# Attention values with the exponentials stationary and V moving, in a kernel of chunk-selected attention and routed experts

## The reference

```python
ub = np.sum(np.maximum(q[:, :, :, None, :] * k_min[:, :, None, :, :], q[:, :, :, None, :] * k_max[:, :, None, :, :]), axis=-1)
ub = np.where(causal, ub, -1000000000.0)
top_chunks = np.argsort(ub, axis=-1)[..., -top_k:]
scores = scale * np.matmul(q, k.transpose(0, 1, 3, 2))
...
mask = sel & (pos[:, None] >= pos[None, :])
scores = np.where(mask, scores, -1000000000.0)
attn = np.exp(scores - np.max(scores, axis=-1, keepdims=True))
attn = attn / (np.sum(attn, axis=-1, keepdims=True) + 1e-09)
out = np.matmul(attn, v)
...
logits = x @ w_gate
expert_idx = np.argmax(logits, axis=1)
for e in range(E):
    ...
        keep = np.argpartition(-gw, capacity)[:capacity]
        tok_idx = tok_idx[keep]
    h = np.maximum(x[tok_idx] @ w1[e], 0.0)
    out[tok_idx] = gate_w[tok_idx, None] * (h @ w2[e])
```

## Time and profile before

| what | value |
|---|---|
| runs | 266.33, 266.83, 269.99 us; median 266.83 |
| profiled execution | 266.53 us |
| its span, first to last instruction | 264.8 us |
| granted clock of PE over the span | 1.00 (the 2.4 GHz level) |
| busy PE, DVE, ACT, POOL | 256.2, 213.2, 149.6, 211.3 us |
| pairs 0 to 15 and what leads up to them | up to about 222 us of the span |

### The profile page before, as it was taken

How to read it: one execution, slowest core, us unless ns; L and a number is a source line. 1 busy time by engine, 2 the same in 40 slices (tenths; PEclk the granted TensorE clock), 3 DMA queues, 4 the chain that set the end, 5 groups by cost and what they waited for, 6 DMA issues and landing times.

```text
span 264.8 us, 9133 instructions
## 1 busy us (share of the span) xinstructions
PE 256.2 (97%) x3824; PEld 164.4 (62%) x3824; DVE 213.2 (81%) x582; ACT 149.6 (56%) x227; POOL 211.3 (80%) x280
## 2 busy tenths in 40 slices
PE   7799999999999999999999999999999999989993
PEld 7366566666666566666665666656665657676763
DVE  6886696778989988867889889899999998983332
ACT  2295656565667564647584546564856665873320
POOL 6068889998999899897989898979899971726872
PEclk9999999999999999999999999999999999999999
DMA  9989989999799989997999999999799996941782
GB/s 147 189 145 149 235 225 261 228 187 224 125 208 180 209 145 195 173 219 125 215 160 215 171 190 164 215 162 324 142 207 184 328 212 142 165 103 40 136 167 91
DMA packets 148616, 48.34 MB, mean 183 GB/s; under 512 B 131583, under 2 KB 138870, under 8 KB 148512
## 3 DMA queue, kind: packets, MB, share of 16 engines
q1 hardware_dynamic: 135504, 28.73, 54.1%
q0 software_dynamic: 9936, 18.64, 38.6%
q10 hardware_dynamic: 3136, 0.39, 1.0%
HBM read 57.03 MB, written 11.01 MB: 257 GB/s over the span
## 4 chain that ended last, share of the span: by engine, by line
PE 91%; DVE 3%; ACT 2%; DMA 1%; issue 1%; ACTq 1%; POOL 0%; DVEq 0%
PE OB L637 28%; PE SC L546 27%; PE SC L567 7%; PE OB L1395 4%; PE MM L673 4%; PE SC L1369 4%; PE MM L650 3%; PE OB L721 2%; PE MM L474 2%; PE SC L474 2%; PE MM L513 2%; DMA qn<-in_q_dram 1%; ACT EXB L576 1%; PE MM L712 1%; PE MM L982 1%
## 5 line engine op out<-in xcount | busy, mean ns | idle before, releaser
L576 ACT ACTIVATE EXB<-SC 128x1024 f32<-128x1024 f32 (+1 forms) x87 | 83.1, 966 | 35.6 <-PE SC L546 23.9
L602 POOL TENSOR_TENSOR ES<-ES,EXB 128x512 f32<-128x512 f32 (+1 forms) x81 | 84.4, 1044 | 5.1
L546 PE MATMUL SC<-qT,kT 64*128 64x512 f32 (+3 forms) x476 | 86.3, 464 | 0.1
L637 PE MATMUL OB<-EXB,vn 128*64 128x256 f32 (+3 forms) x704 | 72.9, 361 | 0.0
L637 PEld LDWEIGHTS OB<-EXB,vn 128*64 128x64 f32 x704 | 46.1, 137 | 24.0 <-issue 10.4
L546 PEld LDWEIGHTS SC<-qT,kT 64*128 64x128 f32 x476 | 39.2, 187 | 15.8 <-issue 11.5
L602 POOL TENSOR_TENSOR ES<-EXB 128x512 f32<-128x512 f32 (+1 forms) x29 | 45.3, 1561 | 2.4
L586 POOL TENSOR_SCALAR_AFFINE_SELECT EXB<-EXB 128x256 f32<-128x256 f32 x79 | 34.9, 452 | 5.0 <-ACT EXB L576 5.0
L645 ACT ACTIVATE oT<-OB 128x512 f32<-128x512 f32 (+1 forms) x32 | 15.7, 490 | 40.1 <-PE OB L637 40.1
L567 PE MATMUL SC<-unsT,ind 64*128 64x256 bf16 (+5 forms) x238 | 35.6, 295 | 0.1
L567 PEld LDWEIGHTS SC<-unsT,ind 64*128 64x128 bf16 x238 | 11.8, 95 | 15.9 <-issue 7.1
(11 more groups left out here) (270 smaller groups left out, 405.0 us busy)
## 6 DMA issues: line engine op xcount, KB each, us to landing
w1s<-in_moe_w_dram POOLq DMA_DIRECT2D x8, 1024.0 KB, 8.6
w2s<-in_moe_w_dram POOLq DMA_DIRECT2D x7, 1024.0 KB, 13.9
vn<-in_v_dram SPq DMA_DIRECT2D x32, 192.0 KB, 4.5
kn<-in_k_dram SPq DMA_DIRECT2D x62, 96.0 KB, 3.2
qn<-in_q_dram SPq DMA_DIRECT2D x62, 96.0 KB, 3.5
out_dram<-w1s SPq DMA_DIRECT2D x2, 1536.0 KB, 7.2
out_dram<-out_dram SPq DMA_DIRECT2D x2, 1536.0 KB, 9.8
x_rows<-xp SPq DMA_DIRECT2D x7, 384.0 KB, 3.9
```

The lines of the kernel that those rows point to most:

```text
L546: op("pe", lambda: pe.matmul(o, kT[j][pr, ts(kt)], qT[j][pr, q0:q1], start=not flags and (not cols or cols[0] == 0), stop=bool(flags)), r= ...
L576: op("act", lambda: ac.activation(Ex(st, None, 0, W), src, ACTF.Exp, scale=SCALE), r=pk, w=[f"E{st}"])
L602: op(e, lambda: sy.queue[e].tensor_tensor(o, in0, in1, ALU.add), r=[f"E{s2}", f"E{first[0]}"] if first else [f"E{s2}"] + kt, w=kt)
L637: op("pe", lambda: pe.matmul(OB[pr, q0:q1], vn[s][:, kt, h, :], ex, start=(n == 0), stop=last), r=[f"vn{s}{h}", "ES0" if st is None else f ...
```

## The change

In `values` the operands change places. A 128x64 half of a block of exponentials is stationary, in the left or right column half of PE's array (u = 0, 1), and V moves, with a 65th column of ones. One pair takes 84 matmuls of 65 columns (21 blocks, two heads, two halves). The output comes out as rows, 64 numbers and the denominator for each head, so the folds, the sums with ones, oT for the pairs before the last, and the 12 transposes go.

A new `rows_out(i - 1)` on DVE at the start of pair i adds 1e-9, takes reciprocals, scales the rows from OB into RN, and transposes RN in 32x32 squares into RT. POOL copies RN to xp, and xp is written out once in a batch. The gate logits are made from RT by eight matmuls (`logits`), behind the bounds, or behind the first two score steps at kk=0 of a live batch and in pair 15 (`turn`). ACT copies them, POOL adds them up over the batch in LGA, and `logits_sum` adds the parts on PE. Counts, tables and the sort's product go to OB instead of MM.

Expert weights are loaded in quarters, 52 of them in pairs 1 to 13, four in a pair, between the scores. `sort_rank` moves from the end of pair 11 to pair 12, behind `rows_out`. The gate weights come in five DMAs, four of them for a layout in oT that `logits` needs.

```diff
-                def fold(st, e="gp", i=0):
...
-                def own_fold(i):
...
+                def values(i):
                     s = i % NB
...
+                    blocks = [(st, kt, q, c + q * 128 - q0) for st in ((0, 1, 2, 3, 5, 4) if short(i) else range(6))
+                              for kt, q0, q1, c in STEPS[st] for q in range(q0 // 128, q1 // 128)]
...
+                        for h in range(2):
+                            o = q // 3 * 512 + (q % 3 * 2 + h) * (D + 1)
+                            for u in range(2):
+                                op("pe", lambda: pe.matmul(OB[u * 64:u * 64 + 64, o:o + D + 1], Ex(st, h, c + u * 64, 64), vn[s][:, kt, h, :],
...
+                def rows_out(i):
...
+                    op("dve", lambda: ve.tensor_scalar(rb, so, 1e-9, None, ALU.add), r=["O0", "O1"], w=[rk])
+                    op("dve", lambda: ve.reciprocal(rden[:], rden[:]), r=[rk], w=[rk])
+                    op("dve", lambda: ve.tensor_tensor(RN.rearrange("p (a b c) -> p a b c", a=2, b=NT), xi, rx, ALU.mult), r=["O0", "O1", rk], w=["RN"])
+                    op("dve", lambda: ve.transpose(RT, RN), r=["RN"], w=["RT"])
+                    op("gp", lambda: gp.tensor_copy(xp[:, :, p, :], RN.rearrange("p (t c) -> p t c", t=NT)), r=["RN"], w=[f"xp{p}"])
...
+                def logits(i):
+                    p = i % NPB
+                    for j in range(4):
+                        for u in range(2):
+                            o = (M0, MBf)[u][j * 32:j * 32 + 32, 0:192]
+                            x = bass.AP(ES, u * 64 * 2 * S + S + j * 32, [[2 * S, 64], [128, NT], [1, 32]])
+                            op("pe", lambda: pe.matmul(o, WB[u * 64:u * 64 + 64, p, j, :], x, start=True, stop=True),
...
-                                op("pe", lambda: pe.matmul(MBf[c * 32:c * 32 + 32, o * 32:(o + hi - lo) * 32], ohb[:, jt, :], Cv[:, :, c, :],
+                                op("pe", lambda: pe.matmul(OB[c * 32:c * 32 + 32, 512 + o * 32:512 + (o + hi - lo) * 32], ohb[:, jt, :], Cv[:, :, c, :],
...
+                    if i and i < NP - 1:
+                        rows_out(i - 1)
+                        wparts(i, 0)
+                    if i == 12:
+                        sort_rank()
                     if i == NP - 1:
                         sort_rows(True)
-                        vw_mm()
-                        clear_xg("k", 0)
-                    if i:
-                        sums(i - 1)
-                        scale_lg(i - 1)
-                        if short(i):
-                            scale_rows(i - 1)
+                    turn = live and kk == 0 or i == NP - 1
+                    if turn:
+                        logits(i - 1)
+                        logits_take(i - 1)
                     if i:
                         folds(i, 0, 1)
+                        wparts(i, 1)
...
                     if i + 1 < NP:
                         bounds(i + 1)
+                        if i and not turn:
+                            logits(i - 1)
+                            logits_take(i - 1)
```

More of the change, by code:

```diff
@@ L245, in _body @@
                 kn = [al(pers, "kn", [128, NT, 2, D]) for _ in range(NB)]
-                vn = [al(pers, "vn", [128, NT, 2, D]) for _ in range(NB)]
+                vn = [al(pers, "vn", [128, NT, 2, D + 1]) for _ in range(NB)]
                 qT = [al(pers, "qT", [128, S]) for _ in range(2)]
@@ L414, in _body, with wload, wkeys, wparts @@
                 WG = ["wg0", "wg1"]
[L416 to L422, removed]
+                WBK = ["Wb0", "Wb1", "Wb2", "Wb3"]
+                def wload(e, part, after=(), js=range(4)):
+                    for j in js:
+                        key = [f"w{part + 1}_{e}" if j == 0 else f"w{part + 1}_{e}{j}"] + (["LGA"] if part and e == E - 2 else [])
+                        if part == 0:
+                            src = bass.AP(moe_w1.tensor, moe_w1.offset + e * Dm * Fd + j * 128 * Fd, [[Fd, 128], [1, Fd]])
+                            dst = w1s[e][:, j, :]
+                        else:
+                            src = bass.AP(moe_w2.tensor, moe_w2.offset + e * Fd * Dm + j * 256 * Dm, [[2 * Dm, 128], [1, 2 * Dm]])
+                            dst = w2s[e][:, 2 * j:2 * j + 2, :].rearrange("p b c -> p (b c)")
+                        op("gpd", lambda: gp.dma_start(dst, src), r=list(after), w=key, dsem=f"d_w{part + 1}_{e}")
+                def wkeys(e, part):
+                    return [f"w{part + 1}_{e}"] + [f"w{part + 1}_{e}{j}" for j in (1, 2, 3)]
+                def wparts(i, n):
+                    for m in {0: (0,), 1: (1,), 2: (2, 3)}[n]:
+                        if 0 < i < NP - 2:
+                            w = (i - 1) * 4 + m
+                            wload(w // 8, w // 4 % 2, (), (w % 4,))
                 def tables():
@@ new lines, in logits_take, with logits_sum @@
+                def logits_take(i):
+                    src = bass.AP(MM, 0, [[1024, 128], [512, 2], [1, 192]])
+                    if i % NPB == 0:
+                        op("act", lambda: ac.activation(LGA, src, ACTF.Copy), r=["M0", "MB"], w=["LGA"])
+                        return
+                    op("act", lambda: ac.activation(LGT, src, ACTF.Copy), r=["M0", "MB"], w=["RT"])
+                    op("gp", lambda: gp.tensor_tensor(LGA, LGA, LGT, ALU.add), r=["RT", "LGA"], w=["LGA"])
+                def logits_sum(i):
+                    for c in range(4):
+                        op("pe", lambda: pe.matmul(OB[c * 32:c * 32 + 32, 0:192] if i < NP - 1 else M0[c * 32:c * 32 + 32, 0:192], SEL[:, c % 2, :], LGA[:, c // 2, :], start=True, stop=True),
+                           r=["LGA", "Sel0", "Sel1"], w=[lgk(i)], inc=(c == 3))
+                    x = OB if i < NP - 1 else M0
+                    op("dve", lambda: ve.transpose(x[:, 192:384], x[:, 0:192]), r=[lgk(i)], w=["lgT"])
@@ L1085, in keep_warm @@
                            r=["ident_bf", "ind0", "ind1"], w=[k], inc=False)
-                def short_warm():
-                    for n in range(12):
-                        pr = slice(n % 2 * 64, n % 2 * 64 + 64)
-                        op("pe", lambda: pe.matmul(M0[pr, 0:65], ident_f[:, pr], ident_f[:, 0:65], start=True, stop=True),
-                           r=["ident_f"], w=["M0"], inc=False)
-                warm(52, 152)
+                warm(111, 64)
                 take_k(0, 0)
@@ L1155, in _body @@
                             select(i, st)
-                        fold(1, "dve")
-                        fold(2, "dve")
-                    if live and kk == 0:
-                        gate_in(bb)
                     if live and kk == 1:
@@ L1203, in _body @@
                         take_k(i + 2)
-                    own_fold(i)
                     if i == 1:
@@ L1231, in _body @@
                         merge(bb)
+                        rows_out(i)
                         vw_turn()
@@ L1289, in _body @@
                 last_row()
[L1290 to L1291 removed]
+                last_values((0,), (3, 9))
+                last_values((1,))
                 last_low(3, "act")
```

308 lines of the change are left out of this document (124 added, 184 removed), and 3 rows, old and new, of the table ADDS.

## The result

The changed kernel takes 300.2 us (median of four runs, 297.4 to 304.0) against 268.4 for the kernel before. The ratio is taken from the faster executions of each (297.4 and 297.9 against 266.3 to 270.0): 1.112, interval 1.092 to 1.132. I had forecast 263.1, within 257 to 270. The profiled execution took 297.4 us, with a span of 295.6.

The account below looks back on a forecast made before the run. PE was taken as the bound, busy 97% of a 264.8 us span. Pairs 1-3 -1.8, kk=0 +1.2, kk=1 -0.75, kk=2 -1.2, kk=3 -1.2, startup +0.3: 266.53 - 3.45 = 263.1 us, range 257 to 270.

Parts of the forecast that it names:

- 58 forecast: Value matmuls on PE: 58 ns each, 84 a pair, 4.87 us against 4.59 before.
- rival D: Value matmuls don't stream, as stationary tiles change 84 times a pair; 279 us at 70 ns each; chance 0.12.
- 0.6 forecast: Ordinary pairs 1 to 3: each gains 0.6 us, after 0.25 given back to waits for ACT's exponentials.
- the kk=1 pairs: Pairs 5, 9, 13: ACT's exponent pass between exponentials costs 0.4 us more, leaving a gain of 0.25 each.
- rival C: DVE's queue ahead of rows_out doesn't shrink, so PE stalls longer at kk=2 and kk=0; 269.1 us; chance 0.13.
- My 0.4 for that stall: kk=2 pairs: PE's wait for RN before the counts, once DVE's diagonal comparison shrinks; 0.7 us was then taken.
- The step that failed: POOL's work: folds go, four quarter issues a pair and one cast come; claimed hidden, no one's bound.
- Tail ... 0: Tail after the last sums: PE loses six transposes of pair 14 but then waits for DVE's gate; 0 us.
- My last sentence: Signs of being wrong: PE waits for RT before the logits in every pair, or quarters late for the expert stage.
- Up to pair 1: Startup: five gate-weight loads instead of two delay SP's next q loads; at most 2.1 us, 0.3 taken.
- kk=0 pairs: Pairs 4, 8, 12: logits wait for RT and their sum is added; 0.4 us slower each.
- kk=2 pairs: Pairs 6, 10, 14: sums and transposes go, counts wait for OB; a gain of 0.4 us each.

Follow-up runs that it names:

- e2: e1 with all 52 weight quarters issued behind pair 15's last sums, none in the pairs; read for its pairs only: pair 15 starts at 214.19 us.
- e4: e1 with the weights moved to the ends of pairs 2, 4, 6, 8, 10, 12 and 13, still issued as quarters; ratio 1.041 to the kernel before.
- e11: e1 with the weight quarters starting in pair 3 instead of pair 1; ratio 1.072 to the kernel before.
- e8: The kernel before with only the weights changed, to 52 quarters from pair 1 on at the changed kernel's places; ratio 1.088.
- e12: e9 with whole 128x128 blocks of exponentials stationary, 42 value matmuls a pair instead of 84; one run, 334.8 us.
- e10: e9 with 12 to 32 of a pair's value matmuls moved ahead of the last two score steps; 292.3 to 297.9 us.
- e1: The changed kernel with the key LGA kept on only the first of the four w2_6 quarters in pair 15; ratio 1.089 to the kernel before.
- e9: e1 with weights as single 1 MB loads at the ends of pairs 2 to 13 and four gate loads moved later on SP; ratio 1.041 to the kernel before.
- the shifted run: The changed kernel with 47 startup fillers of 150 columns instead of 111 of 64, PE's program 128 instructions shorter ahead of pair 0; no time given.
- run 59: Not a follow-up run: the words are part of a sentence saying that matmuls with stationary halves follow one another 59 ns apart.

## Why the prediction was wrong

**What held: the engine work.** Values took 4.95 us a pair (212.58 to 217.53), 59 ns a matmul, against 58 forecast. So rival D, the slower one, was not what made it slower. In e2 pairs 2 and 3 gained 0.64 and 0.56, pair 1 0.33 (0.6 forecast), the kk=1 pairs 0.21 (0.25), pairs 7 and 11 0.51 (0.6). On DVE the diagonal comparison shrank as read from the tail's rows, 0.28 and 0.82 us where I had 0.28 and 0.80 and before 1.20 and 1.31:

```profile
100.79 0.28 DVE L841 TENSOR_TENSOR w2s<-w2s,G 128x128 bf16<-128x128 f32 x1
101.11 0.82 DVE L841 TENSOR_TENSOR w1s<-w2s,G 128x640 bf16<-128x640 f32 x1
```

The counts then waited 0.5 us at most in e2, within the bounds, so rival C was not it either. (My 0.4 for that stall does not follow from my own times, 94.2 - 93.46, which give 0.7, or 1.1 with the 0.37 of the transposes taken off as well; I then took 0.7.) That these two shrank as POOL's folds went is what the Trainium skill's page "SBUF — State Buffer", section "Who interferes with whom", leads one to expect of a locked port pair; no run here separates the port from POOL's other effects.

**The step that failed** is "POOL loses its folds and gains four quarter issues a pair and one cast: hidden, it is no one's bound". I costed the quarters' issues on POOL and not what the transfers meet. Of the 30.8 us between the spans, 19.5 lie ahead of pair 15, and 18.9 of them vanish when no weights move in the pairs (233.1 to 214.2, e2):
- V late in pairs 3 and 4, with the clock's fall behind it: 15.96 + 20.04 against 12.52 + 14.63 in e2, 8.9 us. By e4 and e11 the early start is the cause. Why SP's issues of Q and K (pieces of 128 bytes) slow down then was not tried.
- PE's code late, the other 10 us: nine pauses of 9.5 us and the one of 1.2 under DVE's name, where e2 has one of 1.4.

**The term I didn't have** is PE's own code. I priced 84 matmuls instead of 24 by stream and load, and by a filler row of twelve, 48 instructions with their loads, which is too short to run out of code. An ordinary pair now takes 548 instructions of PE instead of 348, and 336 of them in 5 us. (The 670 and 480 in the expectations are the whole program divided by 16.) A block of 256 lasts 3.7 us there, and 5.4 to 11.8 in the pairs of the kernel before, wherever the count begins. It is the density together with other traffic, the weights' above all: e2 (dense, no weights) has one pause of 1.4 us, e8 (weights, not dense) and e12 (half the value instructions, with weights) have none. How much density it takes stays open: with the values split, e10 still pauses 6.6 us.

**"Tail ... 0"** was wrong by 11.3 us. I read the transposes out of the tail and passed over the quarters of w2_6, whose common key makes POOL wait three times 3.5 us with the gathers queued behind. My last sentence names quarters late for the experts as a sign of being wrong, but gives them no price. e1 gives 6.5 of it back. Of the 4.8 left in e1, 3.7 are idle time of PE (8.8 us in that stretch against 5.1 before; the longest waits are 1.7 for the gathers and 1.0 for ACT) and 1.1 are busy time, at a mean clock of 0.96; the cause of those waits stays open.

**Sizes.** Up to pair 1 it took 1.0 more where I took 0.3. kk=0 pairs +1.14 (pair 4), +0.68 (pair 8) and +1.52 (pair 12, with the one pause) in e2, where I took +0.4. kk=2 pairs gained 0.17 (pairs 6 and 10), not 0.4. The sort's move, which I didn't price, cost no wait. With these and the pause, e2 reaches pair 15 at 214.2, 0.6 later than before, where my sum had 210.2: without weights in its way, and the pause of 1.4 taken off, the change gains some 0.9 us up to there, not 3.4. No version here beats the kernel before; the best are e4 and e9 at 1.041.

## What to carry to other kernels

Count instructions as well as columns: where one engine turns to many short matmuls, ask how long a block of its code lasts and what else the DMA queues carry meanwhile. Splitting a load into pieces moves its issues into another queue and its bytes into another stretch of time; read both queues, and look at each piece's write keys, since a shared key makes pieces wait for one another. A gain of PE time per pair is safe only while nothing that was covered by that time (code, V, the clock) comes due.

## What I had not expected of the hardware

PE's code arrives in packets of 16 KB, about 256 instructions, and under load PE stood up to 3.5 us at their ends (in the shifted run), each time until 1.3 to 1.6 us after a packet had landed; the profile books this as "issue", or under a semaphore, as DVE's 1.2 us in pair 10. Stationary halves in the two column halves of the array run 59 ns apart where a whole block takes 227 (2 x 113), so two halves cost half as much as one whole. With idle times of 1.1 and 2.8 us for V, the granted clock fell to the 1.2 GHz level, and PE's next matmuls took up to half as long again (7.57 us against 5.0). The pauses of up to 2.0 us in pairs 5 to 14 brought no fall: it stayed at 1.00 from 87.5 to 255.5.
